# A gated unit in the banks of x, sums halved over two units in two tiles only, and four steps of the second tile moved to other units

## What is computed

```python
qn = q / (norm(q, axis=1) + 1e-6);  kn = k / (norm(k, axis=1) + 1e-6)     # over the tokens
a = softmax(kn.T @ qn / tau)                                              # 256 x 256
x = v @ a                                                                 # 6016 x 256
xn = x / sqrt(mean(x * x, axis=-1) + 1e-6) * rms_g
g = xn @ w_gate                                                           # 256 x 1536
y = (g * sigmoid(g) * (xn @ w_val)) @ w_out                               # 1536 x 256
h = y @ w_in                                                              # 256 x 2048
out = (h - tanh(h)) @ w_out2                                              # 2048 x 256
```

## Time and profile before

| | |
|---|---|
| median of 3 runs | 1193.73 us (1192.22 to 1194.16) |
| profiled execution | 1193.26 us, of which the span is 1191.3 |
| TensorE busy | 1179.2 us (99%) |
| VectorE busy | 855.7 us (72%) |
| ScalarE busy | 366.4 us (31%) |
| GpSimd busy | 27.1 us (2%) |
| mean granted TensorE clock | 0.998 |

### The profile page before, as it was taken

How to read it: one execution, slowest core, us unless ns; L and a number is a source line. 1 busy time by engine, 2 the same in 40 slices (tenths; PEclk the granted TensorE clock), 3 DMA queues, 4 the chain that set the end, 5 groups by cost and what they waited for, 6 DMA issues and landing times.

```text
span 1191.3 us, 15906 instructions
## 1 busy us (share of the span) xinstructions
PE 1179.2 (99%) x5315; PEld 983.2 (83%) x5315; DVE 855.7 (72%) x1447; ACT 366.4 (31%) x587; POOL 27.1 (2%) x19
## 2 busy tenths in 40 slices
PE   8999999999999999999999999999999999999998
PEld 7878788888888888888888888888888888888998
DVE  5797866767667687586596676766868659658666
ACT  6765621411321321231141142132123123113121
POOL 4400000000000000000000000000000000000000
PEclk9999999999999999999999999999999999999999
DMA  9515011001002002001001100100200100100100
GB/s 345 212 58 155 1 18 18 1 16 20 0 0 35 0 0 35 0 0 30 5 0 18 18 0 10 25 0 0 35 0 0 31 0 0 18 1 1 18 1 14
DMA packets 105210, 33.91 MB, mean 28 GB/s; under 512 B 92384, under 2 KB 100832, under 8 KB 105184
## 3 DMA queue, kind: packets, MB, share of 16 engines
q1 hardware_dynamic: 103952, 32.95, 10.9%
q10 hardware_dynamic: 1232, 0.62, 0.2%
HBM read 27.40 MB, written 6.16 MB: 28 GB/s over the span
## 4 chain that ended last, share of the span: by engine, by line
PE 89%; DVE 5%; ACT 2%; DMA 2%; issue 1%; SPq 0%; DVEq 0%; ACTq 0%
PE ring L942 51%; PE out_acc L958 18%; PE y_acc L958 16%; PE out_acc L926 2%; DMA qk_in<-in_q_dram 2%; DVE h_lo L746 1%; DVE act L742 1%; ACT act L477 1%; PE y_acc L872 1%; DVE h_hi L836 1%; PE y_acc L883 1%; DVE wl_lo L580 0%; SPq L321 0%; PE ring L1037 0%; PE y_acc L926 0%
## 5 line engine op out<-in xcount | busy, mean ns | idle before, releaser
L477 ACT ACTIVATE act<-ring 128x512 f32<-128x512 f32 (+1 forms) x333 | 196.5, 590 | 711.1 <-PE ring L942 681.6
L746 DVE TENSOR_TENSOR h_lo<-act,h_hi 128x512 fp32r<-128x512 f32 (+1 forms) x336 | 228.7, 681 | 10.7
L733 DVE TENSOR_TENSOR act<-ring,act 128x512 f32<-128x512 f32 (+1 forms) x141 | 95.0, 674 | 144.5 <-ACT act L477 144.5
L742 DVE TENSOR_TENSOR act<-ring,act 128x512 f32<-128x512 f32 (+1 forms) x192 | 129.2, 673 | 82.4 <-ACT act L477 80.8
L958 PE MATMUL out_acc<-h_hi,wl_hi 128*128 128x512 f32 (+1 forms) x384 | 149.5, 389 | 1.5 <-DVE h_lo L746 0.9
L958 PE MATMUL out_acc<-h_lo,wl_hi 128*128 128x512 f32 (+1 forms) x384 | 147.7, 385 | 0.0
L958 PE MATMUL out_acc<-h_hi,wl_lo 128*128 128x512 f32 (+1 forms) x384 | 147.7, 385 | 0.0
L942 PE MATMUL ring<-y_hi,wl_lo 128*128 128x512 f32 (+1 forms) x384 | 147.7, 385 | 0.0
L942 PE MATMUL ring<-y_hi,wl_hi 128*128 128x512 f32 (+1 forms) x384 | 147.7, 385 | 0.0
L942 PE MATMUL ring<-y_lo,wl_hi 128*128 128x512 f32 (+1 forms) x384 | 147.6, 384 | 0.0
L836 DVE CAST h_hi<-act 128x512 fp32r<-128x512 f32 (+1 forms) x308 | 129.7, 421 | 12.9
(11 more groups left out here) (154 smaller groups left out, 1599.6 us busy)
## 6 DMA issues: line engine op xcount, KB each, us to landing
out_dram<-out_rows SPq DMA_DIRECT2D x88, 64.0 KB, 1.8
qk_in<-in_k_dram SPq DMA_DIRECT2D x9, 512.0 KB, 9.4
qk_in<-in_q_dram SPq DMA_DIRECT2D x9, 512.0 KB, 10.6
v_in<-in_v_dram SPq DMA_DIRECT2D x72, 64.0 KB, 2.2
w_in<-in_moe_w_out_dram SPq DMA_DIRECT2D x14, 256.0 KB, 2.9
w_in<-in_moe_w_in_dram SPq DMA_DIRECT2D x8, 256.0 KB, 3.2
w_in<-in_moe_w_gate_dram SPq DMA_DIRECT2D x6, 256.0 KB, 5.8
w_in<-in_moe_w_val_dram SPq DMA_DIRECT2D x6, 256.0 KB, 6.7
```

What stands on the lines that cost most here:

```text
L477: nc.scalar.activation(act[:, u % RING, 0:width], bank(name)[:, 0:width], func).then_inc(act_ready, 1)
L733: nc.vector.tensor_tensor(buf, bank(gate)[:, 0:width], buf, ALU.mult).then_inc(bank_free, 1)
L742: nc.vector.tensor_tensor(buf, bank(hidden)[:, 0:width], buf, ALU.subtract).then_inc(bank_free, 1)
L746: nc.vector.tensor_tensor(h_lo[:, u % RING, 0:width], act[:, u % RING, 0:width], f32(h_hi[:, u % RING, 0:width]), ALU.subtract).then_inc(h ...
```

## The change

- **The end of a sum.** `finish_down` halves over the last two units (`HALVED`), and in the first and last tile only. In all other tiles every unit is multiplied into half 0 and half 1 in turn; half 0 counts as complete after the last unit's half 0.
- **Hidden units begun at once**: two instead of three in the first and last tile (`BEGUN`).
- **The third raw unit.** In tile 0 the gate and value products of unit 2 go into the two banks of `x0_acc` (`LENT`) and wait for `x_copied` instead of `bank_free`.
- **The first x.** ScalarE multiplies both halves by g straight from `x0_acc`, then squares both, each after VectorE's low part of that half (`u_ready`), then copies both. VectorE makes the low parts straight from `x0_acc` and squares nothing.
- **The second x** is taken after unit 8 of the gated units (`TAKE_AT`) and no longer after the sum y.
- **The last three weight blocks** are split at hidden units 4, 6 and 8 and no longer at 1, 3 and 5.

```diff
-HIDDEN_BEGUN = 3
+HALVED = 2
+BEGUN = 2
+TAKE_AT = 8
@@
-    LATE = {u: EARLY + n for n, u in enumerate((2, 3, 4, 5, 6, 7, 8, 9, 10, 11, G + 1, G + 3, G + 5))}
+    LATE = {u: EARLY + n for n, u in enumerate((2, 3, 4, 5, 6, 7, 8, 9, 10, 11, G + 4, G + 6, G + 8))}
@@
+        LENT = (("gate", KC), ("value", KC))
-        def bank(name):
+        def bank(name, t=None):
+            if t == 0 and name in LENT:
+                return x0_acc[:, LENT.index(name), :]
             return ring[:, ORDER[name] % RING, :]
@@ ScalarE, first x
             for d in range(KC):
                 act_e.wait_ge(x_full, d + 1)
+                nc.scalar.mul(u_hi[:, d, :], x0_acc[:, d, :], g_c[:, d:d + 1]).then_inc(u_hi_ready, 1)
+            for d in range(KC):
+                act_e.wait_ge(u_ready, d + 1)
+                nc.scalar.activation(squares[:, d, :], x0_acc[:, d, :], ACT.Square).then_inc(sq_ready, 1)
+            for d in range(KC):
                 nc.scalar.copy(xt[:, d, :], x0_acc[:, d, :]).then_inc(x_copied, 1)
-                act_e.wait_ge(x_copied, d + 1)
-                nc.scalar.mul(u_hi[:, d, :], xt[:, d, :], g_c[:, d:d + 1]).then_inc(u_hi_ready, 1)
-            nc.scalar.activation(squares[:, 1, :], xt[:, 1, :], ACT.Square).then_inc(sq_ready, 1)
@@ ScalarE, tile 0
                     if f in LATE:
                         split_block(LATE[f])
+                    if f == TAKE_AT:
+                        take_x(1, TILE)
                 cast_unit(G - 1, ("value", G - 1))
                 sum_y(0, TILE)
-                take_x(1, TILE)
@@ VectorE, first x
-            dve.wait_ge(x_copied, 1)
-            nc.vector.tensor_tensor(squares[:, 0, :], xt[:, 0, :], xt[:, 0, :], ALU.mult).then_inc(sq_ready, 1)
-                nc.vector.scalar_tensor_tensor(out=u_lo[:, d, :], in0=xt[:, d, :], scalar=g_c[:, d:d + 1],
+                nc.vector.scalar_tensor_tensor(out=u_lo[:, d, :], in0=x0_acc[:, d, :], scalar=g_c[:, d:d + 1],
@@ TensorE
+                if isinstance(t, int) and t == 0 and name in LENT:
+                    pe.wait_ge(x_copied, LENT.index(name) + 1)
+                    return
@@
                     for d in range(KC):
                         ins = down_half(kind, f, d, u, units, acc)
+                        if f == units - 1 and d == 0:
+                            ins.then_inc(full, 1)
                     ins.then_inc(h_used, 1)
@@
-                    for f in range(units - LAG, units):
+                    halved = HALVED if first or last else 0
+                    for f in range(units - LAG, units - halved):
+                        down(kind, f, u + f, units, acc, full)
+                    for f in range(units - halved, units):
                         pe.wait_ge(h_ready, t * U + (u + f + 1))
                         ins = down_half(kind, f, 0, u + f, units, acc)
-                    ins.then_inc(full, 1)
-                    for f in range(units - LAG, units):
+                        if f == units - 1:
+                            ins.then_inc(full, 1)
+                    for f in range(units - halved, units):
                         down_half(kind, f, 1, u + f, units, acc).then_inc(h_used, 1)
@@
-                begun = HIDDEN_BEGUN if first or last else 1
+                begun = BEGUN if first or last else 1
```

More of the change, by code:

```diff
@@ L774, in raw_gate @@
                 dve.wait_ge(scale_step, SCALE_STEPS)
-                nc.vector.tensor_tensor(act[:, f, :], bank(("gate", f)), scales[:, :],
+                nc.vector.tensor_tensor(act[:, f, :], bank(("gate", f), 0), scales[:, :],
                                         ALU.mult).then_inc(bank_free, 1)
@@ L781, in raw_value @@
                     dve.wait_ge(unit_ready, f - KC + 1)
-                nc.vector.tensor_tensor(scaled_value[:, f % KC, :], bank(("value", f)), scales[:, :],
+                nc.vector.tensor_tensor(scaled_value[:, f % KC, :], bank(("value", f), 0), scales[:, :],
                                         ALU.mult).then_inc(bank_free, 1)
@@ L941, in up_half @@
                     for w_part, part in PASSES:
-                        ins = nc.tensor.matmul(bank(name)[:, 0:width], weights(c, w_part),
+                        ins = nc.tensor.matmul(bank(name, t if first else None)[:, 0:width], weights(c, w_part),
                                                (hi if part else lo)[:, c, 0:width],
@@ L962, in down_half, with down @@
                     return ins
-                def down(kind, f, u, units, acc):
+                def down(kind, f, u, units, acc, full):
                     if first and f % (BLOCK // C) == 0:
@@ L1010, in tile @@
                                 pe.wait_ge(y_ready, t * KC)
-                        down("down", late, late, G, y_acc)
+                        down("down", late, late, G, y_acc, y_full)
                 finish_down("down", 0, G, y_acc, y_full)
@@ L1030, in tile @@
                                 pe.wait_ge(out_turned, t * KC)
-                        down("down2", f - LAG, G + f - LAG, H, out_acc)
+                        down("down2", f - LAG, G + f - LAG, H, out_acc, out_full)
                 finish_down("down2", G, H, out_acc, out_full)
```

## The result

| | before | after |
|---|---|---|
| median of 6 runs each | 1193.72 us (1192.22 to 1195.13) | 1188.47 us (1188.0 to 1189.78) |
| ratio | | 0.9957, 95% interval 0.9945 to 0.997 |
| profiled execution, span | 1193.26, 1191.3 us | 1188.0, 1185.9 us |
| start phase, up to the first gated product | 63.89 us | 64.10 us |
| tile 0, from there to the first product of tile 1 | 97.10 us | 94.73 us |

The span lost 5.4 us: 2.37 in tile 0 and 3.32 in the middle tiles, while the last tile is 0.10 longer and the start phase 0.21. Stages with the same order repeat to some 0.04 us from run to run; the one exception is 0.17 us more in the ten middle tiles of the run with the order in tile 0 alone.

What follows compares the result with a forecast made beforehand. TensorE fills the span, so only its waits could be won: 3.2 + 0.4 + 1.15 + 0.45 + 0.38 + 0 - 0.1 = 5.5 us, from 1193.73 to 1188.2 us. The forecast's own bounds were 1187 to 1189.4 us.

Steps and rivals of the forecast that it cites:

- part 1: Middle tiles, sums no longer halved: TensorE's wait at each tile's end goes, 3.2 us, bounds 0 and 3.4.
- part 2: First tile's start, first x and lent banks: sum of squares 0.4 us earlier, 0.4 us together, bounds 0.27 and 0.45.
- part 3: First tile's middle: waits at last gated unit and first output product shrink, 1.0 us, bounds 0.5 and 1.2; restarts 0.15.
- restarts: First tile, behind the waits at the last gated unit and first output product: 0.15 us for the restarts that follow.
- part 4: First tile's later work: moving splits removes the wait at 135.99, 0.45 us; halving two units the one at 157.34, 0.38 us.
- part 5: Last tile: waits at y and first output product cancel, 0; first transpose 0.17 us later, less up to 0.2; taken as -0.1.
- (b): Middle tiles: the wait doesn't go, not being for the order of products; 2.3 us remain, 1191.4 us; chance 0.09.
- (c): Middle tiles: y comes too late for the first hidden product; a 4.4 us handover makes it slower, 1196.1 us; chance 0.03.
- (d): First tile: the lending wins its own 0.43 us besides, 1187.8 us; chance 0.77 counted together with the forecast.
- with that gone and with three more products ahead: First tile's first output product: early second x and more products ahead make hidden unit 0's low part ready at 120.7, turn 120.76.
- (a): First tile: handovers of y cost more than the old order's rows show; 1.6 us lost, 1189.8 us; chance 0.11.

## Why the prediction was right

The forecast was 1188.2 us, and 1188.47 was measured. Since the medians scatter by more than its terms, the terms are compared by stages.

| term | forecast | measured |
|---|---|---|
| part 1, middle tiles | 3.2 | 3.32 |
| part 2, up to the first product with x | 0.4 | 0.47 |
| part 3, from there to the first output products | 1.0 | 0.88 |
| rest of tile 0 (restarts 0.15, part 4 0.45 and 0.38) | 0.98 | 1.02 |
| part 5, last tile | -0.1 | -0.10 |
| start phase (nothing forecast) | 0 | -0.21 |
| sum | 5.5 | 5.4 |

**Part 1** was right in its place, its mechanism and its size, 0.35 us in each of nine tiles and 0.17 in the tenth. The run with that line alone shows it, and the rival "the wait doesn't go" (b) is excluded by it. Rival (c) did not come about with 1.9 us to spare, and the run with 0.91 us of cover shows the price that it would have had.

**Part 2** came out 0.02 above its upper bound. The mechanism is the one forecast: the sum of squares now waits for ScalarE's second square (63.75 in the rows of tile 0), and tile 0 behind it is earlier by as much. The lending wins nothing of its own, without the earlier x and with it; rival (d) is excluded. The low parts of u read PSUM in the changed kernel, and the two took 0.75 and 0.74 us (1.41 together, since the second starts before the first ends), while each of those from the ordinary memory took 0.75: the longer fixed term for a PSUM source, which the prediction weighed from the Trainium skill, "VectorE: DVE Perf Modes", isn't seen here either.

**Part 3** was right in its sum and wrong in its reason. The step "with that gone and with three more products ahead" took the early second x for one of two causes. Alone it leaves that wait as it was, and undone in the changed kernel it costs 0.01 us. What ended the idle time before the first tanh was TensorE: also before the change. The prediction counted the operations ahead of the tanh and did not read what it waited for. That the sum held all the same was luck as to this cause: the products ahead carried it alone. The cause is the order alone, and there two effects: the last gated unit's wait goes (0.74 us with its restart), and y's half 1 and with it the first hidden unit are complete earlier, since two units are begun on half 0 and not three. The new wait for y was forecast to end at 115.15, with 0.04 us between the low part and the product. It is 0.15 us, here and in the last tile (the last section shows when), so the wait in tile 0 costs 0.42 us with its restart and the gain is 0.88 instead of 1.0. That is rival (a) in its mechanism, at less than a tenth of its price.

**Part 4.** With the later splits, the wait at 135.99 of the earlier trace rows goes and the one at the tile's end stays; with the order alone it is the other way round. So both terms have the causes that the prediction named, the first as far as the three splits, which moved together, can show it: 0.64 us (0.45 and the 0.15 of restarts were foretold), and in the run with the order alone tile 0 is 0.37 us shorter behind its first output product, where 0.38 was foretold.

**Part 5.** The two waits at y and at the first output product cancel but for 0.11 us (42.35 us to the second output product, 42.24 before). The first transpose is 0.28 us later, where 0.17 was foretold, and the time behind the last issue is 0.20 shorter, where up to 0.2 was. The 0.11 us at y, and the 0.11 by which the first transpose is later than foretold, are once more the 0.15 in the place of 0.04. That the stage came out at -0.10 all the same was in part luck: 0.17 us less some 0.07 had been put in, and 0.28, with 0.02 of longer issues, less 0.20 were measured. The fixed 2.0 us of the Trainium skill, "DMA: Bandwidth & Descriptors", section "Anatomy of one DMA", stands there for transfers that GpSimd issues, which the prediction leaves out. Those here come from SyncE and ScalarE, and the span ended 1.89 us behind the last issue before and 1.69 after. That the end goes by the first transpose and not by the second is shown by the run with the old order in the last tile: the second transpose is later there, and the end earlier.

## What to carry to other kernels

Halving a sum to hand it over early needs something that waits for it; where other products already cover the handover (here 1.8 us, eight products of 512 columns), it only takes the cover from the last unit's low part. An engine's operations ahead of a late result are no cause until the row of that result says what ended its idle time: here it was TensorE, and moving them won nothing. When a queue's issues set the end, sharing them out wins only until the DMA engines are full.

## What was not expected of the hardware

Up to the first gated product, the changed kernel and the seven kernels made from it by edits behind that point have the same code, and it took them 63.67 to 64.64 us (each read from its profiled run), while the ten middle tiles took 951.42 or 951.43 in the seven of these with the same code there. This scatter alone is larger than most terms of the sum. A product that waits for another engine's result starts 0.05 us behind it in some places (before: the low part of the last unit) and 0.15 in others (y's low part of half 0, and the first output product); the one behind it follows after 0.34 or 0.31 us (512 columns). So from the end of the result to the second product it takes 0.39 or 0.45 us.

What goes with the one and the other is the number of waits that the code has right in front of the product. Behind two or more in a row (`bank_free` and `y_ready` for y's low part of half 0; `x_copied`, `w_ready` and `h_ready` for the first output product of tile 0) the trace has a wait instruction of its own, an EVENT_SEMAPHORE of 0.05 us, ahead of the product's weight load. In the changed kernel y's low part counts as there at 114.87, this instruction (L1003) starts at 114.90, the weight load at 114.98 and the product at 115.01. Behind a single wait there is no such instruction: where y is halved over three units, the low part of half 1 is there at 116.09 and weight load and product start at 116.13. From tile 0 on, the fourteen traces have 170 products that follow the one ahead by over 0.27 us because they wait for a result. The 70 with the extra instruction start 0.135 to 0.136 us behind their result, the 100 without it 0.043 to 0.045. No run changed the number of waits and nothing else, so this is read from the traces and not tested. It means that a late product behind several waits costs 0.06 us more up to the next product, and it is what the prediction missed: it took its 0.04 from products behind one wait.
